# Clustered attention with two expert layers on one core: score tiles two units apart, and the second head's rows loaded and clustered beside the first's

## What is computed

```python
q_assign = np.argmax(np.einsum('bhsd,hcd->bhsc', q_n, c_n), axis=-1)
k_assign = np.argmax(np.einsum('bhsd,hcd->bhsc', k_n, c_n), axis=-1)
mask = q_assign[:, :, :, None] == k_assign[:, :, None, :]
scores = np.where(mask, scale * np.matmul(q, k.transpose(0, 1, 3, 2)), -1e9)
attn = np.exp(scores - np.max(scores, axis=-1, keepdims=True))
out = np.matmul(attn / (np.sum(attn, axis=-1, keepdims=True) + 1e-9), v)
```

## Time and profile before

| | |
|---|---|
| median of three runs | 973.36 us (973.28 to 974.22) |
| profiled execution | 974.71 us, of which 973.0 from the first instruction to the last |
| PE, DVE, ACT, POOL busy | 908.8, 528.2, 421.9, 136.5 us |
| mean granted clock of PE | 0.975 of full |
| attention | the first 315 us or so |
| feed-forward layer and experts | the rest |

### The profile page before, as it was taken

The page is one execution under the profiler, slowest core; times in us unless marked ns, Lnnn a source line. Parts: engine busy times, 40 slices in busy tenths (PEclk is TensorE's granted clock), DMA queues, the critical chain, the costliest instruction groups (busy, mean ns, idle before and its releaser), DMA issues.

```text
span 973.0 us, 12424 instructions
## 1 busy us (share of the span) xinstructions
PE 908.8 (93%) x4299; PEld 733.0 (75%) x4299; DVE 528.2 (54%) x950; ACT 421.9 (43%) x684; POOL 136.5 (14%) x144
## 2 busy tenths in 40 slices
PE   3889999999999999999999995599999999999995
PEld 2666777667676888888888884488888888888884
DVE  6468878778775543446443644244353444435373
ACT  2457676776767422434234322224343442434320
POOL 2012112212211100000400131400000000004062
PEclk9999999999999999999999997599999999999998
DMA  3213314314216333232532351435342634527364
GB/s 86 66 41 92 116 42 114 95 49 118 84 57 221 130 109 107 87 130 88 173 127 89 119 173 70 148 138 178 107 162 86 205 114 150 179 95 250 127 217 155
DMA packets 84301, 118.98 MB, mean 122 GB/s; under 512 B 19258, under 2 KB 47930, under 8 KB 84256
## 3 DMA queue, kind: packets, MB, share of 16 engines
q1 hardware_dynamic: 79328, 104.08, 33.2%
q0 software_dynamic: 4928, 14.35, 4.2%
HBM read 89.12 MB, written 29.39 MB: 122 GB/s over the span
## 4 chain that ended last, share of the span: by engine, by line
PE 79%; DVE 15%; issue 2%; DMA 1%; ACT 1%; POOL 0%; SPq 0%; POOLq 0%; DVEq 0%; ACTq 0%
PE psum L845 10%; PE psum L846 10%; PE psum L847 10%; PE psum L859 9%; PE psum L860 9%; PE psum L861 9%; PE psum L774 6%; DVE neg_max L1345 5%; PE psum L759 2%; PE psum L990 2%; PE psum L739 2%; PE psum L760 2%; DVE qa L1352 1%; PE psum L857 1%; PE psum L856 1%
## 5 line engine op out<-in xcount | busy, mean ns | idle before, releaser
L774 PE MATMUL psum<-probs,vx 128*128 128x386 f32 x384 | 158.7, 495 | 0.3 <-ACT probs L1056 0.3
L859 PE MATMUL psum<-down_hi,hid_hi 128*128 128x512 f32 x384 | 151.3, 394 | 0.0
L861 PE MATMUL psum<-down_hi,hid_lo 128*128 128x512 f32 x384 | 149.8, 390 | 0.0
L860 PE MATMUL psum<-down_lo,hid_hi 128*128 128x512 f32 x384 | 149.8, 390 | 0.0
L1056 ACT ACTIVATE probs<-psum 128x384 f32<-128x384 f32 x192 | 91.9, 491 | 89.4 <-PE psum L760 86.4
L1223 ACT ACTIVATE hid_hi<-psum 128x448 fp32r<-128x448 f32 x64 | 35.0, 547 | 185.5 <-PE psum L847 179.6
L1345 DVE TENSOR_REDUCE neg_max<-psum 128x1 f32<-128x768 f32 x96 | 90.9, 952 | 29.8 <-PE psum L739 29.5
L1629 DVE SCALAR_TENSOR_TENSOR hid_lo<-psum,hid_hi 128x384 fp32r<-128x384 f32 x64 | 35.6, 557 | 124.2 <-ACT hid_hi L1223 113.6
L1197 ACT ACTIVATE gelu<-psum 128x512 f32<-128x512 f32 x48 | 28.7, 599 | 158.8 <-PE psum L847 151.1
L845 PE MATMUL psum<-sx_hi,up_hi 128*128 128x448 f32 x256 | 94.7, 370 | 0.0
L846 PE MATMUL psum<-sx_lo,up_hi 128*128 128x448 f32 x256 | 94.4, 369 | 0.0
(11 more groups left out here) (189 smaller groups left out, 1500.5 us busy)
## 6 DMA issues: line engine op xcount, KB each, us to landing
raw<-in_moe_w SPq DMA_DIRECT2D x64, 512.0 KB
raw<-in_moe_w_in SPq DMA_DIRECT2D x24, 512.0 KB
raw<-in_moe_w_out SPq DMA_DIRECT2D x24, 512.0 KB
slot_x<-zeros SPq DMA_DIRECT2D x7, 1024.0 KB, 5.4
raw_q<-in_q SPq DMA_DIRECT2D x32, 192.0 KB, 3.3
raw_k<-in_k SPq DMA_DIRECT2D x32, 192.0 KB, 3.6
slot_rows<-slot_x SPq DMA_DIRECT2D x8, 768.0 KB
slot_y<-y_sb SPq DMA_DIRECT2D x7, 768.0 KB, 3.8
```

What stands on the lines that cost most here:

```text
L774: mm(psum[:, 5 + half, 0:WIDE], vx[:, n % 2, c], probs[:, at % SLOTS], start=(c == 0), stop=(c == J - 1)).then_inc(unit_done, 1)
L859: mm(dst, hid_hi[:, f % 2, cols], down_hi[:, slot, f % GP], start=(f == 0), stop=False)
L860: mm(dst, hid_hi[:, f % 2, cols], down_lo[:, slot, f % GP], start=False, stop=False)
L861: return mm(dst, hid_lo[:, f % 2, cols], down_hi[:, slot, f % GP], start=False, stop=(f == pieces - 1))
```

## The change

Six things are done. PE's head(n) issues tiles 0 and 1 of head n+2 at units 8 and 10, tiles 2 to 5 of head n+1 at units 1, 3, 5 and 6 (before: 9, 11 and 0, 2, 4, 6), the similarity at unit 3 and not 1, and the one-hots' turn in front of tile 5. DVE's list follows: the reduction of tile 0 stands in front of head_result(n, 0), the similarities behind that of tile 3, the one of tile 1 in front of the rows. ACT's first pair_hi moves from unit 2 to 1. Head 1's rows are loaded into the still empty staging buffer of the weights, raw1, directly behind head 0's, with a semaphore of their own, and head 2's rows take the place of head 1's in the queue. Head 1 is turned into clusters beside head 0, with its similarity in bank 4. The table load of ACT moves to the front, and first_cluster_rows is gone: ACT makes both copies for head 0 too. first_head is rewritten on PE, ACT and DVE so that head 0 carries the pieces that every other head carries.

```diff
...
@@ -341,7 +342,7 @@
         prep = {}
-        for use in ("sim 0", "turn 0", "max 0", "sim 1", "turn 1", "sim 2", "turn 2", "max 1"):
+        for use in ("sim 0", "turn 0", "turn 1", "max 0", "sim 2", "turn 2", "max 1"):
             prep[use] = len(prep)
@@ -363,6 +364,12 @@
+        def raw_rows(m):
...
+            if m == 1:
+                return tuple(raw1[:, x].rearrange("p c f -> p (c f)")[:, 0:S] for x in range(2))
+            return raw_q[:], raw_k[:]
...
         def own(n):
@@ -413,9 +420,10 @@
-                for dst, src in ((raw_q, q_h), (raw_k, k_h)):
+                for dst, src in zip(raw_rows(n), (q_h, k_h)):
                     for half in range(2):
-                        sp.dma_start(dst[half * D:(half + 1) * D], src[n]).then_inc(qk_in, DMA)
+                        sp.dma_start(dst[half * D:(half + 1) * D], src[n])\
+                            .then_inc(qk_first_in if n == 1 else qk_in, DMA)
@@ -423,9 +431,10 @@
             load_rows(0)
+            load_rows(1)
             load_values(0)
             sp.wait_ge(rows_lo, 2)
-            load_rows(1)
+            load_rows(2)
             load_values(1)
@@ -441,9 +450,8 @@
-            for m in (2, 3):
-                sp.wait_ge(rows_lo, 2 * m)
-                load_rows(m)
+            sp.wait_ge(rows_lo, 6)
+            load_rows(3)
             sp.wait_ge(zeros_set, 1)
@@ -708,15 +716,16 @@
-                pe.wait_ge(prep_free, prep[f"sim {m}"])
+                if m != 1:
+                    pe.wait_ge(prep_free, prep[f"sim {m}"])
                 for w, rows in enumerate((qb, kb)):
...
                         at = (w * J + j) * 2 * C
-                        last = mm(psum[:, 7, at:at + 2 * C], rows[:, m % SLOTS, j * P:(j + 1) * P],
+                        last = mm(psum[:, 4 if m == 1 else 7, at:at + 2 * C], rows[:, m % SLOTS, j * P:(j + 1) * P],
                                   cen_r[:].rearrange("p b h t c -> p (b h t c)")[:, m * 2 * C:(m + 1) * 2 * C],
                                   start=True, stop=True)
-                last.then_inc(prep_ready, 1)
+                last.then_inc(sim_first if m == 1 else prep_ready, 1)
@@ -783,51 +792,55 @@
+                similarity(0)
+                similarity(1)
+                turn_onehot(0)
+                for i in range(5):
+                    scores(0, i)
+                turn_onehot(1)
+                scores(0, 5)
+                turn_max(0, "max 0", J)
+                scores(1, 0)
+                turned(0, 0, 1)
+                turned(0, 1)
                 for u in range(UNITS):
...
                     values(0, u)
-                    if u == 1:
-                        similarity(1)
+                    if u == 0:
+                        scores(1, 1)
+                    elif u == 1:
+                        similarity(2)
+                        scores(1, 2)
                     elif u == 3:
-                        turn_onehot(1)
-                    elif 5 <= u < 9:
-                        scores(1, u - 5)
-                    if u == 5:
-                        similarity(2)
+                        scores(1, 3)
+                    elif u == 5:
+                        scores(1, 4)
+                        turn_onehot(2)
+                    elif u == 6:
+                        scores(1, 5)
                     elif u == 8:
-                        turn_onehot(2)
+                        turn_max(1, "max 1", J)
                     elif u == 9:
-                        scores(1, 4)
-                        scores(1, 5)
-                        turn_max(1, "max 1", J)
-                    elif u >= 10:
-                        scores(2, u - 10)
+                        scores(2, 0)
+                    elif u == 11:
+                        scores(2, 1)
...
                     values(n, u)
-                    if n + 1 < HEADS:
-                        if u in (0, 2, 4, 6):
-                            scores(n + 1, 2 + u // 2)
-                        elif u == 8:
-                            turn_max(n + 1, f"max {n + 1}", J)
-                    if n + 2 < HEADS:
-                        if u == 1:
-                            similarity(n + 2)
-                        elif u == 6:
-                            turn_onehot(n + 2)
-                        elif u in (9, 11):
-                            scores(n + 2, (u - 9) // 2)
...
-            similarity(0)
-            turn_onehot(0)
-            for i in range(J):
-                scores(0, i)
-            turn_max(0, "max 0", J)
-            turned(0, 0, 1)
-            turned(0, 1)
+                    if u == 6 and n + 2 < HEADS:
+                        turn_onehot(n + 2)
+                    if u in (1, 3, 5, 6) and n + 1 < HEADS:
+                        scores(n + 1, 2 + (1, 3, 5, 6).index(u))
+                    elif u == 8 and n + 1 < HEADS:
+                        turn_max(n + 1, f"max {n + 1}", J)
+                    if u == 3 and n + 2 < HEADS:
+                        similarity(n + 2)
+                    elif u in (8, 10) and n + 2 < HEADS:
+                        scores(n + 2, (u - 8) // 2)
...
             first_head()
@@ -1019,6 +1032,7 @@
             copy(cen_s[:, 1:2], cen_s[:, 0:1], ACT.Sqrt).then_inc(cen_root, 1)
+            nc.scalar.preload_act_table_set(EXP_AND_LN)
             act.wait_ge(cen_tr, 1)
@@ -1026,12 +1040,16 @@
-                act.wait_ge(qk_in, (m + 1) * (4 * DMA))
+                raw_q, raw_k = raw_rows(m)
+                if m == 1:
+                    act.wait_ge(qk_first_in, 4 * DMA)
+                else:
+                    act.wait_ge(qk_in, max(m, 1) * (4 * DMA))
                 if m >= SLOTS:
...
                 if w == 0:
-                    copy(qa[:, s], raw_q[:], ACT.Copy).then_inc(rows_hi, 1)
+                    copy(qa[:, s], raw_q, ACT.Copy).then_inc(rows_hi, 1)
                 else:
...
@@ -1106,15 +1119,20 @@
+                rows(0, 0)
+                rows(0, 1)
+                rows(1, 0)
+                rows(1, 1)
+                rows(2, 0)
+                cluster_rows(0)
+                rows(2, 1)
+                cluster_rows(1)
+                exps(0, 0)
                 for u in range(UNITS):
                     next_exps(0, u)
-                    if u == 4:
-                        cluster_rows(1)
-                    elif u in (5, 6):
-                        rows(2, u - 5)
+                    if u == 6:
+                        reciprocals(0, 0)
                     elif u == 7:
-                        reciprocals(0, 0)
-                    elif u == 9:
                         cluster_rows(2)
@@ -1125,8 +1143,8 @@
                         reciprocals(n - 1, 1)
-                    elif u in (2, 4) and n % 2 == 0:
-                        pair_hi(n - 1, u // 2 - 1)
+                    elif u in (1, 4) and n % 2 == 0:
+                        pair_hi(n - 1, u // 4)
                     elif u == 6:
...
@@ -1304,25 +1315,30 @@
-                a, b, coef, raw = ((qa, qb, split_q, raw_q), (ka, kb, split_k, raw_k))[w]
+                a, b, coef = ((qa, qb, split_q), (ka, kb, split_k))[w]
                 s = m % SLOTS
...
                 dve.wait_ge(rows_hi, 2 * m + w + 1)
-                dv.scalar_tensor_tensor(out=b[:, s], in0=a[:, s].bitcast(F32), scalar=coef[:], in1=raw[:],
+                dv.scalar_tensor_tensor(out=b[:, s], in0=a[:, s].bitcast(F32), scalar=coef[:], in1=raw_rows(m)[w],
                                         op0=ALU.mult, op1=ALU.add).then_inc(rows_lo, 1)
...
-                dve.wait_ge(prep_ready, prep[f"sim {m}"] + 1)
-                both = psum[:, 7, 0:4 * J * C].rearrange("p (j t c) -> p j c t", t=2, c=C)
-                dv.tensor_reduce(sim[:], both, AX.X, ALU.add).then_inc(prep_free, 1)
+                both = psum[:, 4 if m == 1 else 7, 0:4 * J * C].rearrange("p (j t c) -> p j c t", t=2, c=C)
+                if m == 1:
+                    dve.wait_ge(sim_first, 1)
+                    chain.link(dv.tensor_reduce(sim[:], both, AX.X, ALU.add))
+                else:
+                    dve.wait_ge(prep_ready, prep[f"sim {m}"] + 1)
+                    dv.tensor_reduce(sim[:], both, AX.X, ALU.add).then_inc(prep_free, 1)
...
                 full = (P, 2 * J, C)
-                dve.wait_ge(prep_free, prep[f"sim {m}"] + 1)
+                if m != 1:
+                    dve.wait_ge(prep_free, prep[f"sim {m}"] + 1)
                 chain.link(dv.tensor_reduce(best[:], sim[:], AX.X, ALU.max))
...
@@ -1391,22 +1401,29 @@
+                rows(0, 0)
+                rows(0, 1)
                 rows(1, 0)
+                similarities(0)
                 rows(1, 1)
+                clusters(0)
                 similarities(1)
+                rows(2, 0)
                 clusters(1)
-                rows(2, 0)
+                for i in range(J):
+                    row_max(0, i)
+                max_to_rows(0, "max 0", 0, J)
+                row_max(1, 0)
```

(41 more changed lines are left out.)

## The result

The changed kernel takes 947.67 us (946.98 to 948.24, four runs) against 973.38: a ratio of 0.9728 with a 95% interval of 0.9717 to 0.9740. 948.0 was forecast, within 944 to 957. The profiled execution took 948.05, its span is 946.3. That the median lies within 0.4 of the forecast is partly luck: by the spans of the two profiles the gain is 26.7 us where 25.5 had been summed, and it is 25.7 by the medians only because the profiled execution lay 1.3 above the median before and 0.4 above it now.

The account below looks back on a forecast made before the run. PE's own work plus its stalls on DVE's reductions was taken to bound the attention stage. Terms 1.9 - 12.0 - 15.4 = -25.5 us took 974.71 to 949.2, less 1.35 to the median: 947.9, rounded 948.0; range 944 to 957.

Parts of the forecast that it names:

- The floor of a head: Steady heads: PE's own work, summed from single pieces of a stretch without stalls, takes 16.43 us per head.
- DVE in step: Steady odd heads: DVE finishes each piece at least 0.35 us before PE asks, so the head runs at PE's 16.43.
- Even heads: Steady even heads: recip beside POOL delays tile 4's reduction to the edge; priced 0.3 us each, ends 0 and 1.3.
- Rival B: Even heads: DVE's three long forms (recip, kb, hit) appear at once, costing 1.3 us per head; 955 us, chance 0.24.
- The start: Up to mark 0, DVE's step closing head 0's first preparation: +1.9 us, ends +0.5 and +4.5.
- even sharing: Start's eight row loads: if the second four share evenly with the first, head 0's rows come +2.6 us late; 0 taken.
- Head 0: From mark 0 to mark 1: 17.8 us against 29.84, six us of it at half matmul pace; -12.0.
- The fourteen intervals: Mark 1 to 15: thirteen steady intervals 215.4 us plus a last of 14.7, together 230.1 against 245.56; -15.4.
- Behind mark 15: After the last preparation mark: same code, weight loads move with head 13's last unit; no change expected.
- Rival D: Tile 0 at unit 8 waits for ACT's late cluster rows, blocking PE's queue; slower, 982 us if 3.2 late; chance 0.05.
- Rivals C and E: C: start fails, late rows and longer half pace, 955 us, chance 0.07. E: no gain, feed-forward weights not earlier, 0.02.
- The first theory for the start: Head 0: rows, similarity, clusters and cluster rows of head 1 stood on its path; given for the -12.0 us.

Follow-up runs that it names:

- short_max: Changed kernel with every first-pass reduction over half of the score columns: 944.27 us, 0.9688 of the kernel before.
- dve_list_old: Changed kernel with only DVE's list of the later heads put back to the old order: 967.02 us, 0.9942 of the kernel before.
- pe_list_old: Changed kernel with only PE's list of the later heads put back to the old places: 961.57 us, 0.9868 of the kernel before.
- start_only: Changed kernel with the old head(n) put back on PE, ACT and DVE, keeping the new start: 962.28 us, 0.9871 of the kernel before.
- tile5_first: Changed kernel with tile 5 back in front of the one-hots' turn, one unit behind tile 4: 954.38 us, 0.9796 of the kernel before.
- loads_only: Kernel before with only head 1's rows loaded early into raw1 and head 2's in their place, all orders old: 974.08 us, 0.9998.
- before_no_read: Kernel before with POOL's subtraction for the pairs' low parts replaced by a memset that reads nothing: 969.91 us, 0.9962.

## Why the prediction was right, point by point

**The floor of a head.** 16.43 from single pieces of one stretch; 16.42 measured, and 16.38 with reductions half as wide (short_max). Right, and shown.

**DVE in step.** All deadlines were met in odd heads as laid out: tile 0's reduction starts 1.10 after the mark, and PE's timeline has no idle time there. dve_list_old and pe_list_old show that the deadlines were the condition.

**Even heads.** 0.3 was priced, 0.16 came. The reduction ended on the edge as foreseen. The price compared a restarted tile (0.62) with a smooth one (0.35), but tile 5 stands behind the one-hots' turn, where it takes 0.55 without any wait: the 0.2 of the slower matmul, already in the 16.43, was counted twice. Rival B, three collisions at once, did not come: kb and hit kept their short forms, but for kb in the first even head. For kb that is partly luck. It still falls together with POOL's L592 in the even heads (229.91 and 229.95), and it is POOL that is stretched there, 1.83 for 1.00. The forecast's reason against B, that POOL's work comes in other moments, does not hold for kb.

**The start.** +1.9 against +2.16. What is missing is the second one-hot turn, which was to lie within the reductions: PE does it between two score tiles, DVE idles 0.39 before the last reduction, and the six end at 25.2 and not at 24.9. The load was undersized too, but without effect on the sum: eight loads at the 222 GB/s of the earlier trace rows were to land at 9.7 and landed at 10.42, yet head 0's one-hots were ready at 15.56, where 15.55 had been laid out. Head 0's own rows were not held up: ACT began them at 7.25, before at 7.18; even sharing (+2.6) is refuted.

**Head 0.** -12.0 against -12.67. The mis-sized term is the time at half pace: six us had been taken from the kernel before, in the changed one PE's matmuls double their pace at 30.95, 4.2 us after the first of the turned scores (26.74). That is not the new lists' doing alone. start_only and tile5_first have the same lists in head 0, and PE is idle as long in front of the turned scores (1.05 and 0.40); there the pace doubles only at about 33.0 and head 0 takes 18.0, which would have been -11.8. The forecast lies between the two, and which of them the changed kernel showed is luck.

The kernel before had a second such spell in head 0, behind waits of 1.54 and 0.27 for head 2's rows. In the first one the granted clock reads 1.00, though equal matmuls took 0.32 for 0.18; in the second one it reads 0.50, the lower of the two levels (1.2 for 2.4 GHz):

```profile
24.60:30.70 6.10, 6.10 (x19) 4.87 (x19) 1.95 (x2) 1.97 (x4) 0.00 (x0) 1.00 0.45 118
...
42.00:44.00 2.00, 2.00 (x6) 1.59 (x5) 0.37 (x1) 1.74 (x4) 0.09 (x1) 0.50 0.96 257
```

The forecast took 29.84 as measured and did not look into it. The changed kernel has one spell of 4.2 us; the two of the kernel before last 6.0 and 3.4 (40.6 to 44.0). Half of the difference is an estimate of what the pace gives: 2.6 of the 12.67.

**The fourteen intervals.** -15.4 against -16.35: the six even heads give 0.66 of the difference (0.15 less in five of them, 0.1 more in the first), the last interval and the odd heads about 0.1 each.

**Behind mark 15** nothing moved, as said (674.1 and 674.2). Since the same code took 671.2 to 674.2 in the profiles of all kernels, an agreement to 0.1 is luck, and a shift of up to 3 us could not be told from none. Rival D (tile 0 blocked by ACT's cluster rows) did not occur: in the odd head of 208 to 224 us ACT's copies end 0.7 before PE's turn, and 0.8 had been worked out. Rivals C and E fell with the table above.

**The first theory for the start,** that the preparation of head 1 stood on head 0's path, is carried by start_only (mark 1 at 43.9 with the old lists of every later head) and loads_only. What is left of the 12.67 beside the pace, some 10 us, is head 1's preparation moved ahead of mark 0 and the waits that went with it; no run separates these two.

## What to carry to other kernels

Where one engine hands small pieces to another through a single buffer, lay both queues out against one time axis, piece by piece from rows of a stretch without a stall, and move both lists together: either list alone made the steady heads longer here. An operation taken off a path pays only when the next one on it is also ready, as the early load showed: nothing alone, 5.2 us with its consumer moved. And two engines that share a port should be ordered by a wait where their start times lie close: here starts 0.03 and 0.05 us apart stretched now the one and now the other.

## What the runs showed that was not expected

The part behind mark 15, whose code is the same in all kernels, took 671.2 us (dve_list_old: span 964.7, mark 15 at 293.51) to 674.2 (the changed kernel) in the profiled executions, with no order that I could find; small differences between whole kernels are therefore read from the marks here. A write-only operation on POOL (0.42 us for 128 x 384, at 152.45 in before_no_read) ran wholly beside DVE's hit and left it at its 0.36, where hit takes 0.78 beside POOL's subtraction, which reads.
